# Two batches' leftover tokens are projected and transposed together in a kernel of attention, gated convolution and spectral mixing

## The chip, the cores and the metric

The kernel runs on one core of a Trainium2 chip. The metric is the device time of one execution in microseconds (us). A core has a matrix engine (TensorE, PE in the profile; its weight loads are the rows PEld), VectorE (DVE), ScalarE (ACT), GpSimd (POOL) and SyncE (SP), which issues the DMA transfers. Each engine runs its own list of instructions in order, and they wait for one another on semaphores.

## The reference

For 4 batches of 576 tokens and width 512 (8 heads of 64):

```python
scores = q @ k.T / 8                       # per head, 576 x 576
kth    = 32nd largest of each row
attn   = softmax(where(scores >= kth, scores, -1e9))
x      = concat_heads(attn @ v)            # 576 x 512

gate = sigmoid(causal 5-tap convolution of x along tokens, per channel)
x    = (gate * (x @ w_val)) @ w_out

u  = x + real(fft over tokens(fft over width(x)))
un = (u - mean(u)) / sqrt(var(u) + 1e-6)   # over the width
out = u + relu(un @ w_ch1) @ w_ch2         # 512 -> 2048 -> 512
```

## The kernel before

**Slots.** Attention is cut into 144 tiles: 4 batches of 4 pairs of heads, 9 tiles of 128 rows of scores to a pair (four to each head, and one that holds the last 64 rows of both). Slot s is one turn of a loop that every engine runs. In it PE makes the scores of tile s, transposes the probabilities of tile s-5 and, in every other slot, multiplies by v (`attend`, tile s-6). DVE finds the 32 largest of each row with eight passes over 576 columns, here called a search: the first half `search(s, 0)` (two MAX8 and two MATCH_REPLACE8) and the second `search(s, 1)` (two and one), for the tiles s-1 and s-2. ACT copies the scores, computes the exponentials of tile s-4 and copies the transposed probabilities.

**Steps.** Everything behind attention is a list of steps for each batch (`STEPS`, L109), which `steps_by_slot` (L160) spreads over the 36 slots that begin at slot 42, 78 and 114, by the costs of `COST`; the last batch has no attention beside it and takes one step a slot from slot 150 on. The steps of a batch are: `val` 0 to 7 (products with w_val; DVE multiplies them by the gate into `gv`), `zed` 2, 0, 1 and `seq` 0 to 2 (the two transforms), `proj` 0 to 4 (product with w_out, one for each tile of tokens; DVE's `make_u` adds the transform and takes mean and variance, GpSimd's `deviation` makes 1/sqrt, DVE's `normalise` makes `un`), `trn` 0 to 4 (PE transposes `un`, ACT copies it twice, as `un_hi` and back into `un`, GpSimd subtracts to get `un_lo`), then `ch0` and `ch1` 0 to 16 (for two groups of tokens: `hidden(f)` and behind it `sums(f-1)`).

**Where a step stands in its slot.** On every engine the first step of a slot's list stands before the second half of the slot's own work, the others behind it. On PE the order is scores, transposes, first step, `attend`, other steps. On DVE it is `search(s, 0)`, first step, `search(s, 1)`, other steps. On ACT the first step stands behind the exponentials, except a `ch0` step below 12.

**Tiles of tokens.** A batch has four tiles of 128 tokens and 64 left over, tile 4. The left over tokens of an even batch lie in rows 0 to 63 of `u[4]`, those of the odd batch behind it in rows 64 to 127. The matmuls of `ch1` take them together in the odd batch (`GROUPS`, L58), and the output is written from there for both. Before the change everything from `proj` 4 to `trn` 4 is done in each batch for itself: in the even batch with 64 rows, and in the odd one the product is made for 128 rows, of which 64 are used.

**Waits that the steps below name.** `zed` 2 waits before each quarter k for the gate products, the last of them for both parts of `val` 7. `project(2)` waits for the copy of `seq` 0, `transpose_un(n)` for `normalise(n)`, `hidden(b, 0, 0)` for `un_lo` of the first two tiles, `sums(b, 0, 0)` for all of `make_u`. The third and fourth buffers of w_ch2 and w_ch1 hold parts of w_out, so SP loads them again only when the last projection is done. In batches 0 and 2 the list puts `val` 6 and 7 into slots 45 and 117, `proj` 0 and 1 into 49 and 121, `seq` 1 and `proj` 2 into 50 and 122, `proj` 3 into 51 and 123, `trn` 0, `trn` 1 and `seq` 2 into 52 and 124, `proj` 4 and `ch0` 0 into 53 and 125. In batch 1, `val` 4 to 6 are in slot 80 and `val` 7 and `zed` 2 in slot 81.

Of the kernel before, what the change touches and what calls it, by code (L numbers as in the profile page):

```python
# [9 lines left out]
ALU = mybir.AluOpType  # L10
# [46 lines left out]

GROUPS = [[[0, 2], [1, 3]], [[0, 2], [1, 3, 4]]]  # L58
# [27 lines left out]

def hidden_bank(b, g, f):

    if g == 0:
        return 3 if f == 1 or f >= 12 and f % 2 == 0 else 2  # L90

    return 2 if (b % 2 == 0 or f == 1) and f % 2 else 3
# [13 lines left out]
TRN_BANK = [3, 2, 3, 3, 3]  # L106
# [9 lines left out]
NORM_AT = {("proj", 1): 0, ("proj", 2): 1, ("ch0", 1): 2, ("ch0", 4): 3, ("ch0", 7): 4}  # L116
COST = {"val": 2.2, "zed": 3.0, "seq": 2.6, "proj": 2.9, "trn": 0.6, "ch0": 3.1}
# [42 lines left out]
def steps_by_slot():  # L160

    out = {s: [] for s in range(ALL_TILES + ATTEND)}
    for b in range(B):
        steps = [(what, b, n) for what, n in STEPS]
# [16 lines left out]
def build(nc, qT, kT, v, w_val, conv_w, w_out, w_outT, w_ch1, w_ch2, feat, cosT, sinT, ident, out):  # L181
    with ExitStack() as ctx:
# [213 lines left out]
        def out_rows(b, r):  # L396

            return slice(0, LEFT) if r == NR - 1 and b % 2 == 0 else slice(0, P)

        def gv_cols(b, r):  # L400
            return slice(ROWS[r][0], ROWS[r][0] + out_rows(b, r).stop)
# [25 lines left out]
        with nc.Block() as block:  # L427

            @block.sync
            def _(sp):  # L430
# [49 lines left out]
                def load_w1(i):  # L480
                    if i % (2 * FC) == NB1 - 1:
                        sp.wait_ge(m_y, NR * (i // (2 * FC) + 1))
                    if i >= NB1:
                        sp.wait_ge(m_h, i - NB1 + 1)
                    sp.dma_start(w1_st[i % NB1][:, :, :, :].bitcast(F32), w1_split[i % FC]).then_inc(m_w1in[i % NB1], 16)

                def load_w2(i):
                    if i % (2 * FC) == NB2 - 1:
                        sp.wait_ge(m_y, NR * (i // (2 * FC) + 1))
# [73 lines left out]
            def _(pe):  # L563
# [129 lines left out]
                def sequence(b, g):  # L693
                    if g == 0:
                        pe.wait_ge(s_resid, 80)
                    elif g == 2:
                        pe.wait_ge(m_u, 2 * NR * b + 4)
# [12 lines left out]
                def project(b, r):  # L710
# [5 lines left out]
                    elif r == 3:  # L716
                        pe.wait_ge(m_u, 2 * NR * b + 2)
                    elif r == 4:
                        pe.wait_ge(m_u, 2 * NR * b + 8)

                    bank = mbank(PROJ_BANK[r])[out_rows(b, r), :]
                    for n, (x, h) in enumerate(((gv_hi, 0), (gv_hi, 1), (gv_lo, 0))):
                        for k in range(KC):
                            for c0, c1, w in w_out_half(b, k, h):
                                mm = pe.matmul(bank[:, c0:c1], x[:, k, gv_cols(b, r)], w, start=n + k == 0,  # L725
# [3 lines left out]
                def transpose_un(b, n):  # L729
                    r = LN[n]  # L730
                    pe.wait_ge(m_un, NR * b + n + 1)
                    if n == 0:
                        pe.wait_ge(m_u, 2 * NR * b + 6)
                    elif n == 1:
                        pe.wait_ge(m_abev, 3 * b + 2)
                    else:
                        pe.wait_ge(m_unT, 2 * (NR * b + n))
                        pe.wait_ge(m_hev, 2 * FC * b + 2)
                    m, at = ROWS[r][1], rows(b, r)
                    bank = mbank(TRN_BANK[n])  # L740
                    for k in range(KC):
                        mm = pe.transpose(bank[:, k * P:k * P + m], un[n % 2][at, k * P:k * P + P], id_sb[at, at])
                    mm.then_inc(m_tr, 1)

                def hidden(b, g, f):
                    i = (2 * b + g) * FC + f
                    if f == 0:
                        pe.wait_ge(m_unlo, NR * b + (NR if g else 2))
# [3 lines left out]
                    if g == 0 and f == 12:  # L752
                        pe.wait_ge(m_unT, 2 * NR * (b + 1))
# [7 lines left out]
                def sums(b, g, f):  # L761
# [3 lines left out]
                    if f == 0 and g == 0:  # L765
                        pe.wait_ge(m_u, 2 * NR * (b + 1))
# [48 lines left out]
            def _(act):  # L815
# [87 lines left out]
                def step(what, b, n):  # L903
# [13 lines left out]
                    elif what == "trn":  # L917
                        m = ROWS[LN[n]][1]
                        act.wait_ge(m_tr, NR * b + n + 1)
                        bank = mbank(TRN_BANK[n]).rearrange("p (k n) -> p k n", k=KC)[:, :, 0:m]  # L920
                        act.activation(un_hi[:, :, un_cols(b, LN[n])], bank, ACT.Copy).then_inc(m_unT, 1)
                        act.activation(un[n % 2][:, 0:KC * m].rearrange("p (k n) -> p k n", k=KC), bank,
# [19 lines left out]
                for s in plan:  # L942
# [7 lines left out]
                    first = any(what == "ch0" and n < 12 for what, b, n in plan[s][0:1])  # L950
# [28 lines left out]
            def _(dve):  # L979
# [94 lines left out]
                def make_u(b, r):  # L1074
                    g = [0, 0, 1, 1, 2][r]
                    at = rows(b, r)
# [28 lines left out]
                def step(what, b, n):  # L1105
                    if what == "val":
# [3 lines left out]
                        if b and n == 0:  # L1110
                            dve.wait_ge(m_y, NR * b)
# [9 lines left out]
                    if (what, n) in NORM_AT:  # L1121
# [22 lines left out]
                for s in plan:  # L1144
                    if due(s, RECIP) and unit_end(s - RECIP) is not None and s - RECIP >= POOL_RECIP:
                        reciprocal(s - RECIP)
                    search(s, 0)
                    for x in plan[s][0:1]:
# [10 lines left out]
                    for x in plan[s][1:]:  # L1159
# [3 lines left out]
            def _(pool):  # L1163
# [180 lines left out]
```

## Time and profile before

| | |
|---|---|
| median of 3 runs | 1044.3 us (1043.85 to 1046.93) |
| the profiled execution | 1048.86 us, of which the span of instructions is 1047.1 us |
| busy: PE, PEld | 965.9 us (92%), 826.2 us (79%) |
| busy: DVE, ACT, POOL | 842.2 us (80%), 645.5 us (62%), 406.9 us (39%) |
| mean granted clock of TensorE | 0.969 |

The profiled execution is one run and 4.6 us above the median. Busy is the union of the spans of an engine's instructions. The ends of matmuls are modelled, so the engine's real pace is read from the starts of its rows, and from the weight loads. A wait is put down to the instruction that came last by the profile.

### The profile page before, as it was taken

What the parts mean: (1) busy time and instruction counts of PE and PEld (TensorE: products, weight loads), DVE (VectorE), ACT (ScalarE), POOL (GpSimd) and SP (SyncE); (2) the same over time, 40 slices, a digit from 0 to 9 for tenths busy, and PEclk for the clock granted to TensorE, in tenths of its full rate; (3) what the DMA queues carried; (4) which work ended last, traced back from release to release, by engine and by line L of the source; (5) the groups of instructions that cost most, each with busy time, mean ns of one, the idle gap of its engine ahead of it and who ended that gap; (6) DMA issues with size and microseconds to landing.
All of it is one profiled execution on the core that took longest, in us unless ns stands there. A gap on an engine that the chain in (4) does not pass through costs nothing.

```text
span 1047.1 us, 20137 instructions
## 1 busy us (share of the span) xinstructions
PE 965.9 (92%) x6784; PEld 826.2 (79%) x6784; DVE 842.2 (80%) x1840; ACT 645.5 (62%) x1421; POOL 406.9 (39%) x543
## 2 busy tenths in 40 slices
PE   4877777899999999989999999989999999999997
PEld 3555566678888898778998898878889887888896
DVE  7999999999999999989999987898999973220000
ACT  5887787965777767556776566666786661132121
POOL 1674554544443333244342333244442222443221
PEclk9997868999999999999999999999999999999999
DMA  8565756550277777401877565410677676069873
GB/s 246 175 197 172 257 175 195 178 191 24 88 284 257 273 271 276 140 18 64 289 262 262 187 219 178 144 34 24 236 255 259 255 253 212 1 227 346 288 247 128
DMA packets 84549, 203.80 MB, mean 195 GB/s; under 512 B 9056, under 2 KB 30304, under 8 KB 84448
## 3 DMA queue, kind: packets, MB, share of 16 engines
q1 hardware_dynamic: 84128, 201.93, 56.6%
q8 instruction: 55, 0.90, 0.4%
q10 hardware_dynamic: 320, 0.59, 0.2%
q14 instruction: 46, 0.38, 0.1%
HBM read 178.89 MB, written 23.59 MB: 193 GB/s over the span
## 4 chain that ended last, share of the span: by engine, by line
PE 59%; DVE 28%; issue 9%; ACT 2%; POOL 1%; DMA 1%; SPq 0%; DVEq 0%; ACTq 0%; POOLq 0%
PE p_m L757 16%; PE p_m L774 15%; DVE rest L1007 13%; DVE top L996 11%; PE p_m L725 5%; PE p_t L605 5%; PE p_t L589 4%; PE p_s L575 4%; PE p_m L616 3%; PE p_m L706 3%; PE p_m L648 2%; DVE gate L1070 1%; DVE gv L1116 1%; PE p_t L609 1%; DMA w_st<-w_split 1%
## 5 line engine op out<-in xcount | busy, mean ns | idle before, releaser
L996 DVE MAX8 top<-rest 128x8 f32<-128x576 f32 x432 | 312.4, 753 | 0.1
L1272 POOL TENSOR_TENSOR hid_lo<-hid,hid_hi 128x256 fp32r<-128x256 f32 (+1 forms) x128 | 107.7, 842 | 299.2 <-ACT hid_hi L932 299.2
L1007 DVE MATCH_REPLACE8 rest<-top,rest 128x576 f32<-128x576 f32 x288 | 216.3, 751 | 0.0
L774 PE MATMUL p_m<-w_st,hid_hi 128*128 128x512 f32 x576 | 181.2, 396 | 3.1 <-DMA w_st<-w_split 1.8
L757 PE MATMUL p_m<-un_hi,w_st 128*128 128x256 f32 (+1 forms) x1024 | 164.3, 303 | 0.0
L838 ACT ACTIVATE s_sb<-p_s 128x576 f32<-128x576 f32 x144 | 93.0, 646 | 98.1 <-PE p_s L575 98.1
L757 PEld LDWEIGHTS p_m<-un_hi,w_st 128*128 128x128 f32 x1024 | 143.5, 188 | 5.6 <-issue 1.9
L931 ACT ACTIVATE hid<-p_m 128x256 f32<-128x256 f32 (+1 forms) x128 | 51.8, 405 | 129.2 <-PE p_m L757 128.3
L589 PE MATMUL p_t<-id_sb,prob 128*128 128x128 f32 x720 | 108.3, 282 | 24.2 <-ACT prob L856 23.9
L605 PE MATMUL p_t<-pT,v_sb 128*64 128x128 f32 (+1 forms) x1600 | 106.6, 284 | 24.3 <-ACT pT L864 24.3
L605 PEld LDWEIGHTS p_t<-pT,v_sb 128*64 128x64 f32 x1600 | 87.5, 146 | 49.0 <-ACT pT L864 30.0
L575 PE MATMUL p_s<-k_hi,q_st 128*128 128x288 f32 x320 | 108.4, 354 | 14.6 <-DVE q_st L1140 8.3
L856 ACT ACTIVATE prob<-prob,bias 128x576 f32<-128x576 f32 x144 | 111.8, 776 | 16.2
L774 PEld LDWEIGHTS p_m<-w_st,hid_hi 128*128 128x128 f32 x576 | 101.1, 188 | 19.8 <-POOL hid_lo L1272 2.2
L774 PE MATMUL p_m<-w_st,hid_lo 128*128 128x512 f32 x288 | 113.5, 394 | 0.0
L589 PEld LDWEIGHTS p_t<-id_sb,prob 128*128 128x128 f32 x720 | 87.1, 144 | 32.4 <-ACT prob L856 30.5
L996 DVE MAX8 top<-s_sb 128x8 f32<-128x576 f32 x144 | 109.7, 762 | 2.9 <-ACT s_sb L838 2.8
L850 ACT ACTIVATE prob<-s_sb,top 128x576 f32<-128x576 f32 x144 | 111.0, 771 | 0.0
L1007 DVE MATCH_REPLACE8 rest<-top,s_sb 128x576 f32<-128x576 f32 x144 | 108.1, 751 | 0.0
L864 ACT ACTIVATE pT<-p_t 128x640 f32<-128x640 f32 x144 | 101.3, 703 | 6.3 <-PE p_t L589 6.3
L1103 DVE TENSOR_TENSOR u<-p_m,u 128x512 f32<-128x512 f32 x18 | 11.5, 685 | 112.9 <-PE p_m L774 112.8
L575 PE MATMUL p_s<-k_lo,q_st 128*128 128x288 f32 x320 | 93.6, 307 | 0.0
(118 smaller groups left out, 1655.8 us busy)
## 6 DMA issues: line engine op xcount, KB each, us to landing
w_st<-w_split SPq DMA_DIRECT2D x256, 512.0 KB, 4.8
w_split<-w_st SPq DMA_DIRECT2D x32, 512.0 KB, 3.4
k_raw<-kT SPq DMA_DIRECT2D x62, 144.0 KB, 3.0
q_raw<-qT SPq DMA_DIRECT2D x60, 144.0 KB, 2.9
u<-w_ch SPq DMA_DIRECT2D x32, 256.0 KB, 4.0
v_sb<-v SPq DMA_DIRECT2D x16, 256.0 KB, 3.0
w_st<-wout_split SPq DMA_DIRECT2D x16, 256.0 KB, 3.9
out<-u SPq DMA_DIRECT2D x16, 256.0 KB, 2.5
```

What stands on the lines that cost most here:

```text
L575: mm = pe.matmul(p_s[:, o, 0:HALF_S], q_st[h][p % 2][:, cols], k[:, o * HALF_S:o * HALF_S + HALF_S], start=n == 0, stop=n == len(parts) - 1)
L589: mm = pe.transpose(p_t[:, c * P:c * P + P], prob[t % 3][:, c * P:c * P + P], id_sb[:, :])
L605: pe.matmul(p_o[D * h:D * h + D, 0, 0:n], v_sb[p % 2][:, c, D * h:D * h + D], pT[tt % 3][:, c, c0:c0 + n], start=c == 0, stop=c == NCH - 1 ...
L757: mm = pe.matmul(mbank(hidden_bank(b, g, f), n), w1_st[i % NB1][:, w, k, :], x[:, k, at:at + n], start=part + k == 0, stop=part + k == KC + 1)
L774: mm = pe.matmul(mbank(j), h[i % 2][:, P * j:P * j + P], w2_st[i % NB2][:, w, :], start=f == 0 and part == 0, stop=f == FC - 1 and part == 2)
L838: act.activation(s_sb[t % NS][:, :].rearrange("p (o n) -> p o n", o=2), p_s[:, :, 0:HALF_S], ACT.Copy, scale=SCALE).then_inc(s_copy, 1)
L850: act.activation(prob[t % 3][:, 0:S], s_sb[t % NS][:, :], ACT.Prelu, bias=kth, scale=-1.0, alpha=1.0 / BIG).then_inc(s_drop, 1)
L856: act.activation(prob[t % 3][:, 0:S], prob[t % 3][:, 0:S], ACT.Exp, bias=bias[t % NK][:, :], scale=-BIG, accum_out=psum_row[:, t % NK:t % ...
L864: act.activation(pT[t % 3][:, :, :].rearrange("p c n -> p (c n)"), p_t[:, 0:SP], ACT.Copy).then_inc(s_pT, 1)
L996: found = dve.max(top[t % NK][:, 8 * n:8 * n + 8], (rest[t % 2] if n else s_sb[t % NS])[:, :])
L1007: chained(dve.match_replace(rest[t % 2][:, :], top[t % NK][:, 8 * n:8 * n + 8], (rest[t % 2] if n else s_sb[t % NS])[:, :], LOWEST), t)
L1272: pool.tensor_tensor(hid_lo[i % 2][:, 0:width(b, g)], hid[:, 0:width(b, g)], hid_hi[i % 2][:, 0:width(b, g)].bitcast(F32), ALU.subtract).t ...
```

## The change

- The even batches have no `proj` 4 and no `trn` 4 any more, and `deviation` and `normalise` of tile 4 are gone there too. `plus_minus` of `seq` 2 writes its result straight into rows 0 to 63 of `u[4]`.
- In the odd batch `make_u` of tile 4 first adds the product of the even batch's 64 rows to them, one DVE operation on 64x512 more. Statistics, deviation, normalising, transposes, copies and `un_lo` of tile 4 are made for all 128 rows there.
- In even batches `trn` 0 stands before `proj` 3, with the two banks of PSUM for `trn` 0 and 1 exchanged. `hidden` alternates its banks from f = 10 instead of 12.
- `deviation` of tile 3 stands behind `un_lo` of `trn` 1 on GpSimd, for all batches, and not at `proj` 3.
- DVE does the first step of a slot ahead of `search(s, 0)` if it is a `val` from 4 on.
- ACT does `ch1` 0 ahead of the exponentials if it is the first step of its slot (slots 66 and 138 after the change).
- The counts of semaphores follow (`us`, `outs`), and SP waits for four projections in an even batch.
- With 56 steps in place of 58, `steps_by_slot` gives the even batches other slots: of batch 0, slot 50 `seq` 1; 51 `proj` 2, `trn` 0, `proj` 3; 52 `trn` 1, `seq` 2; 53 `ch0` 0; 54 `ch0` 1 and 2. Slots 42 to 49 and 71 to 77 keep their steps, and so do all of batch 1 and 3; batch 2 has the pattern of batch 0, 72 slots later.

```diff
-TRN_BANK = [3, 2, 3, 3, 3]
+TRN_BANK = [[2, 3, 3, 3], [3, 2, 3, 3, 3]]
...
+LAST_TILE = [("proj", NR - 1), ("trn", NR - 1)]
+def steps_of(b):
+    if b % 2:
+        return STEPS
+    steps = [x for x in STEPS if x not in LAST_TILE]
+    steps.remove(("trn", 0))
+    steps.insert(steps.index(("proj", 3)), ("trn", 0))
+    return steps
...
 def load_w1(i):
     if i % (2 * FC) == NB1 - 1:
-        sp.wait_ge(m_y, NR * (i // (2 * FC) + 1))
+        sp.wait_ge(m_y, outs(i // (2 * FC) + 1))
...
 def transpose_un(b, n):
-    pe.wait_ge(m_un, NR * b + n + 1)
-    if n == 0:
-        pe.wait_ge(m_u, 2 * NR * b + 6)
-    elif n == 1:
+    pe.wait_ge(m_un, outs(b) + n + 1)
+    if n < 2 and TRN_BANK[b % 2][n] == PROJ_BANK[2]:
+        pe.wait_ge(m_u, us(b) + 6)
+    elif n < 2:
         pe.wait_ge(m_abev, 3 * b + 2)
...
-first = any(what == "ch0" and n < 12 for what, b, n in plan[s][0:1])
+first = any(what == "ch0" and n < 12 or (what, n) == ("ch1", 0) for what, b, n in plan[s][0:1])
...
 def make_u(b, r):
...
     y = mbank(PROJ_BANK[r])
+    at, made = slice(0, P), us(b) + 2 * (r + 1)
+    if r == NR - 1:
+        at, made = rows(b, r), us(b + 1)
+        early = rows(b - 1, r)
+        dve.tensor_tensor(u[r][early, :], y[early, :], u[r][early, :], ALU.add).then_inc(m_u, 1)
...
-    if (what, n) in NORM_AT:
+    if (what, n) in NORM_AT and outs(b) + NORM_AT[what, n] < outs(b + 1):
         normalise(b, NORM_AT[what, n])
...
+    ahead = int(any(what == "val" and n >= KC for what, b, n in plan[s][0:1]))
+    for x in plan[s][0:ahead]:
+        step(*x)
     search(s, 0)
-    for x in plan[s][0:1]:
+    for x in plan[s][ahead:ahead + 1]:
         step(*x)
     search(s, 1)
...
 def plus_minus(b, g):
...
+    if g == 2 and b % 2 == 0:
+        if b:
+            pool.wait_ge(m_put, 16 * puts(b))
+        to = u[NR - 1][at, :]
+        pool.tensor_tensor(to[:, 1:NCOS - 1], a, bb, ALU.subtract).then_inc(m_pm, 1)
+        pool.tensor_tensor(to[:, DM - 1:NCOS - 1:-1], a, bb, ALU.add).then_inc(m_pm, 1)
+        for n in (0, NCOS - 1):
+            pool.tensor_copy(to[:, n:n + 1], ab[at, n:n + 1]).then_inc(m_pm, 1)
+        return
...
-elif what == "proj" and n < NR - 1:
+elif what == "proj" and n < 3:
     deviation(b, n)
 elif what == "trn":
...
+    if n == 1:
+        deviation(b, 3)
```

## Rows read from the trace of the kernel before

**Rows 1.** Stretches: length, busy of PE, PEld, DVE, ACT, POOL, clock, DMA share, GB/s

```profile
232.00:234.00 2.00, 2.00 (x7) 1.63 (x6) 2.00 (x5) 2.00 (x5) 1.29 (x2) 0.50 0.00 0
...
265.00:444.00 179.00, 176.78 (x1396) 154.12 (x1394) 177.48 (x388) 128.85 (x294) 63.91 (x83) 1.00 0.67 231
...
450.00:453.00 3.00, 3.00 (x9) 2.45 (x8) 2.96 (x9) 2.88 (x7) 1.91 (x2) 0.50 0.00 0
...
602.00:660.00 58.00, 58.00 (x405) 51.76 (x404) 45.67 (x97) 37.91 (x82) 17.23 (x19) 1.00 0.57 198
...
971.00:1041.00 70.00, 69.43 (x342) 61.83 (x342) 1.29 (x2) 13.95 (x32) 16.16 (x16) 1.00 0.63 224
```

**Rows 2.** Timeline of PE: start, us, operation [idle before <-releaser]; `zed` 2

```profile
229.85 0.66 PE L682 MATMUL p_m<-wfeat,gv 128*64 128x257 f32 x4 [2.00 <-DVE gv L1116]
...
444.56 0.65 PE L682 MATMUL p_m<-wfeat,gv 128*64 128x257 f32 x4 [0.44 <-DVE gv L1116]
448.13 0.65 PE L682 MATMUL p_m<-wfeat,gv 128*64 128x257 f32 x4 [2.91 <-DVE gv L1116]
...
688.75 1.12 PE L682 MATMUL p_m<-wfeat,gv 128*64 128x257 f32 x4 [2.97 <-DVE gv L1116]
```

**Rows 3.** Timeline of DVE, slots 120 to 123: its idle times (batch 0 has their like)

```profile
704.85 0.15 DVE L1054 TENSOR_SCALAR rinv<-psum_row 128x1 f32<-128x1 f32 x1 [0.47 <-ACT prob L856]
...
708.68 0.43 DVE L1084 TENSOR_TENSOR u<-p_m,pm 128x257 f32<-128x257 f32 x1 [0.69 <-PE p_m L725]
...
713.20 0.43 DVE L1084 TENSOR_TENSOR u<-p_m,pm 128x257 f32<-128x257 f32 x1 [0.80 <-PE p_m L725]
...
720.80 0.43 DVE L1084 TENSOR_TENSOR u<-p_m,pm 128x257 f32<-128x257 f32 x1 [0.64 <-PE p_m L725]
...
723.50 0.55 DVE L1097 TENSOR_SCALAR un<-u,mv,rstd 128x512 f32<-128x512 f32 x1 [0.99 <-POOL rstd L1249]
```

**Rows 4.** Timeline of DVE, slot 81: from its first search pass to `gv`

```profile
444.75 0.76 DVE L996 MAX8 top<-s_sb 128x8 f32<-128x576 f32 x1
...
447.52 0.55 DVE L1116 SCALAR_TENSOR_TENSOR gv<-gate,p_m 128x63 f32<-128x63 f32 x2
```

**Rows 5.** Timeline of DVE, slot 117: its start, second half of search, `gv`

```profile
683.00 0.76 DVE L996 MAX8 top<-s_sb 128x8 f32<-128x576 f32 x1
...
686.11 1.41 DVE L996 MAX8 top<-rest 128x8 f32<-128x576 f32 x2
...
688.15 0.54 DVE L1116 SCALAR_TENSOR_TENSOR gv<-gate,p_m 128x63 f32<-128x63 f32 x2
```

**Rows 6.** Timeline of DVE, slot 125: `make_u` of tile 4 and what follows

```profile
738.55 0.41 DVE L1084 TENSOR_TENSOR u<-p_m,pm 64x257 f32<-64x257 f32 x1
...
740.14 1.38 DVE L996 MAX8 top<-rest 128x8 f32<-128x576 f32 x2
```

**Rows 7.** Groups of instructions, forms apart: xcount, busy us, mean ns, idle before

```profile
L1103 DVE TENSOR_TENSOR u<-p_m,u 128x512 f32<-128x512 f32 x18 | 11.5, 685 | 112.9 <-PE p_m L774 112.8
...
L1097 DVE TENSOR_SCALAR un<-u,mv,rstd 64x512 f32<-64x512 f32 x4 | 3.4, 843 | 10.1 <-POOL un_lo L1263 10.1
```

**Rows 8.** Timeline of PE, slots 124 and 125: `attend`, `trn` 1, `proj` 4, `hidden`

```profile
726.53 1.31 PE L605 MATMUL p_t<-pT,v_sb 128*64 128x128 f32 x20 [0.36 <-ACT pT L864]
...
727.99 0.66 PE L742 MATMUL p_m<-id_sb,un 128*128 128x128 f32 x4
...
732.95 0.48 PE L725 MATMUL p_m<-w_out,un_hi 128*64 128x512 f32 x1
...
735.83 1.11 PE L757 MATMUL p_m<-un_hi,w_st 128*128 128x256 f32 x8
```

**Rows 9.** Timeline of PE: `trn` 4 of batch 2 and the scores behind it

```profile
778.40 0.46 PE L742 MATMUL p_m<-id_sb,un 64*128 64x64 f32 x4
778.79 0.40 PE L575 MATMUL p_s<-k_hi,q_st 128*128 128x288 f32 x1
```

**Rows 10.** Timeline of PE: `val` 6 of batch 2, slot 117

```profile
677.55 1.90 PE L648 MATMUL p_m<-x_new,wslot 128*128 128x257 f32 x8
```

More of the change, by code:

```diff
@@ L85, in un_cols @@
     return slice(c0, c0 + ROWS[r][1])
+TRANSPOSED = [10, 12]
 def hidden_bank(b, g, f):
     if g == 0:
-        return 3 if f == 1 or f >= 12 and f % 2 == 0 else 2
+        return 3 if f == 1 or f >= TRANSPOSED[b % 2] and f % 2 == 0 else 2
     return 2 if (b % 2 == 0 or f == 1) and f % 2 else 3
@@ L163, in steps_by_slot @@
     for b in range(B):
-        steps = [(what, b, n) for what, n in STEPS]
+        steps = [(what, b, n) for what, n in steps_of(b)]
         start = NT * (b + 1) + ATTEND
@@ L394, in folded, with tile_cols @@
             return gate[:, c, o * HALF + P * m:o * HALF + P * m + P]
[L396 to L401, printed above, removed]
+        def tile_cols(r):
+            return slice(ROWS[r][0], ROWS[r][0] + P)
         def w_out_half(b, k, h):
@@ L751, in hidden @@
                         pe.wait_ge(m_hev, hidden_before(i) + 1)
-                    if g == 0 and f == 12:
-                        pe.wait_ge(m_unT, 2 * NR * (b + 1))
+                    if g == 0 and f == TRANSPOSED[b % 2]:
+                        pe.wait_ge(m_unT, 2 * outs(b + 1))
                     at, n = HALF * g, width(b, g)
@@ L917, in step @@
                     elif what == "trn":
[L918 to L922, printed above, removed]
+                        act.wait_ge(m_tr, outs(b) + n + 1)
+                        bank = mbank(TRN_BANK[b % 2][n]).rearrange("p (k n) -> p k n", k=KC)
+                        act.activation(un_hi[:, :, tile_cols(LN[n])], bank, ACT.Copy).then_inc(m_unT, 1)
+                        act.activation(un[n % 2][:, :].rearrange("p (k n) -> p k n", k=KC), bank,
                                        ACT.Copy).then_inc(m_unT, 1)
@@ L1158, in _ @@
                         conv(b, c, part, taps)
-                    for x in plan[s][1:]:
+                    for x in plan[s][ahead + 1:]:
                         step(*x)
@@ L1244, in deviation @@
                 def deviation(b, r):
[L1245 to L1249 removed]
+                    pool.wait_ge(m_mv, outs(b) + r + 1)
+                    pool.tensor_scalar(rstd[:, r, 0:1], mv[:, r, 1:2], EPS_VAR, None, ALU.add).then_inc(m_var, 1)
+                    pool.wait_ge(m_var, outs(b) + r + 1)
+                    pool.tensor_tensor(rstd[:, r, 1:2], rstd[:, r, 0:1], power[:, 0:1], ALU.pow).then_inc(m_rstd, 1)
                 def step(what, b, n):
@@ L1273, in step @@
                                            hid_hi[i % 2][:, 0:width(b, g)].bitcast(F32), ALU.subtract).then_inc(m_hlo, 1)
-                        if g == 0 and n == 1:
+                        if g == 0 and n == 1 and b % 2:
                             deviation(b, NR - 1)
```

64 lines of the change are left out of this document (28 added, 36 removed).

## The prediction

> **What bounds the kernel now.** I read first the busy time by stretch, then every idle time of DVE and of PE in their timelines, and asked at each idle time which of the two had been late. From 230 us on both look full: in 265 to 444 us PE is busy 176.8 of 179 us and DVE 177.5 [rows 1]. The weight loads are busy 154.1 of these 179 us, 86%, against 61.8 of 70, 88%, in the last stretch, where nothing but PE works [rows 1]. So PE really works at nearly its full pace, with DVE as full beside it. PE runs one to two slots ahead of DVE, and that lead lets neither stop for the other except at few places. These places tell which engine the end depends on.
>
> PE stops for DVE before `zed` 2: 2.0 us at 229.9, 0.4 and 2.9 us at 444.6 and 448.1, 3.0 us at 688.8 [rows 2]. It needs the gate products of `val` 6 and 7, and DVE makes them behind its search. DVE stops for PE or for what hangs on PE in the slots of `proj`: 0.47, 0.69, 0.80 and 0.64 us, and 0.99 us for GpSimd's deviation, in batch 2 [rows 3]; batch 0 has the same five within 0.03 us. In 602 to 660 us DVE is busy only 45.7 of 58 us while PE is never idle [rows 1]. So the path to the end goes: DVE up to 230; PE up to the `proj` steps of batch 0; DVE to 448, without an idle time of note; PE through batch 1 to about 659; DVE through `val` to 689; PE from 689 to the end. A saving counts if it lies on this path, on that engine.
>
> **Gate products first.** In slot 81 DVE starts its search at 444.75 and `val` 7 follows at 447.52 [rows 4]. The change puts it in front: 2.77 us earlier. In slots 45 and 117 `val` 6 is the first step and `val` 7 the second; they are now done before `search(s, 0)` and between the halves, so `val` 7 is earlier by the second half, 688.15 - 686.11 = 2.04 us [rows 5]. DVE does the same work in another order. PE gets 2.04 us earlier into `zed` 2 of batches 0 and 2 and, by this part alone, 2.77 us in batch 1.
>
> **DVE in batch 0.** With PE 2.04 us earlier, y of `proj` 0 and 1 and the exponentials come before DVE needs them: the idle times of 0.47, 0.69 and 0.80 us sum to 1.96, less than 2.04. `proj` 2 moves from behind slot 50's search to slot 51, so that DVE reaches it half a search (2.77 us) later, and PE only by a slot's scores and transposes; the idle time of 0.64 goes too. The 0.99 us for the deviation stays. That is 2.60 us of idle time gone from DVE. Of `make_u` for tile 4, 740.14 - 738.55 = 1.59 us go [rows 6]; `normalise` on 64 rows took 0.84 us in the mean of four, on 128 rows 0.55, taken as 0.60 since one of the four was long [rows 3, 7]. Sum for batch 0, on DVE: 2.60 + 1.59 + 0.60 = 4.8 us. With the 2.77 us of slot 81 `zed` 2 of batch 1 starts 7.6 us earlier. PE arrives there 2.04 us earlier and without `proj` 4 and `trn` 4 (2.88 and 0.39 us, below), together 5.3 us. It stood 3.35 us for DVE before [rows 2] and stands 3.35 - 7.6 + 5.3 = 1.1 us now: DVE stays the later one, and what PE saves in this batch is hidden.
>
> **Batch 1.** PE's work is the same but for four transposes with 128 instead of 64 columns, some 0.05 us. DVE has one addition more; the nearest row, on twice the rows and the same columns, took 0.69 us [rows 7]. It lies between 468 and 602 us, where PE leads and DVE's later idle time (12.3 us of 602 to 660 [rows 1]) covers it; were the cover gone, it would cost those 0.69 us, and I keep 0 to 0.7. The 7.6 us are carried to 659.
>
> **Batch 2.** DVE's `val` 7 gives 2.04 us at 689. From there PE's path counts. `proj` 4 took 735.83 - 732.95 = 2.88 us and `trn` 4 0.39 us [rows 8, 9]. That would be 5.3 us, if nothing new makes PE wait. What can is `trn` 1. It waits for `normalise(1)`, which follows `make_u` of `proj` 2, and this now stands in slot 123 behind another first half of a search. Worked out: `normalise(1)` began at 723.50; without the idle times before it (1.96 + 0.64) and with 2.77 us of search and two small operations of 0.15 us [rows 3] more before it, it begins at 723.97 and ends at 724.5. PE's `trn` 1 began at 727.99, so it can start 3.5 us earlier, not 5. Between it and `hidden` lay 7.84 us, of which 2.88 are `proj` 4; `attend`, 1.46 us, which stood before it, now stands behind it [rows 8]. So `hidden(0)` starts at 724.5 + 7.84 - 2.88 + 1.46 = 730.9, 4.9 us earlier than the 735.83 of before, and with `trn` 4 it is 5.3 us. That the two ways agree means that `trn` 1 is nearly just in time: PE waits there 0 to 1 us, and what PE gains more before it is lost in front of it. `hidden(0)` itself needs `un_lo` of `trn` 1: ACT's copies stand behind an exponential, GpSimd's subtraction behind them, by my sum at 728.8, which leaves 2 us. `deviation` of tile 3 behind it hides in GpSimd's idle time, and `normalise` of tile 3 comes five slots later.
>
> **The last batch** has its order. `deviation` out of the way lets `un_lo` come about 1 us sooner, but PE did not wait for it. Its loads of weights start again when `proj` 4 ends, as before, so that stretch moves as one. Cost of the wider `trn` 4 and of the addition: 0 to 0.5 us, taken as 0.1.
>
> **Sum.** 7.6 + 5.3 - 0.1 = 12.8 us off the profiled execution's 1048.86, which gives 1036.1. Off the median of 1044.3 it gives 1031.5.
>
> **A rule against the trace: the clock.** The granted clock is 0.50 in 450 to 453 us, the lower level of 1.2 GHz, behind the waits of 444.6 and 448.1, and in 232 to 234 us behind that of 229.9 [rows 1, 2]; at 688.8 the four matmuls of `zed` 2 took 1.12 us against 0.65 [rows 2]. A low stretch of 3 us costs about 1.5 us against full speed. In batch 1 PE now stands some 1.1 us in place of 3.35. Whether the clock then stays at 2.4 GHz no row decides. The forecast leaves the low stretch in batch 1, and takes no gain in 0 and 2, where DVE or `trn` 1 swallows it.
> The Trainium skill (TensorE: Matmul & The Clock Gate, "What's actually happening") says that the throttled clock is the default and that activity releases it; by it shorter waits would keep the higher level, and the time would be about 1030.0 instead of 1031.5. The trace agrees as far as it shows the low level only behind such waits in this part.
>
> **Rivals.**
> 1. *The clock stays up in batch 1.* For it: the wait shrinks to a third, and PE carries batch 1 alone. Against it: the wait of 2.0 us at 229.9 was enough for a fall. Time: 1031.5 - 1.5 to 2 = 1029.5 to 1030, down to 1027 if other small waits go with it.
> 2. *The even batches get new waits on PE.* `proj` 4 was 2.88 us of PE work between `trn` 1 and `hidden(0)`, which hid the way from `un` through PE, ACT and GpSimd. If my 2 us of slack are not there, PE waits 1 to 3 us in each even batch, and in batch 2 it counts, perhaps with a low clock of 1.5 us behind it: 1033 to 1038.
> 3. *The change gives nothing measurable.* That would be if DVE's order, not PE's work, carried batches 1 and 2 as well. DVE's 12.3 us of idle time before 660 [rows 1] speak against it. Time: within 3 us of 1044.
> 4. *Slower: DVE stands before `val`.* DVE now does a product ahead of its search, and must wait if PE is not done with it; before, 2.77 us of search covered that. Six slots have it (44, 45, 80, 81, 116, 117). If PE has no lead there, DVE stands 2.77 us in each, 16.6 us in all, against 12.8 gained: 1044.3 + 3.8 = 1048. It decides from the point at which PE's product ends later than DVE's slot begins. In slot 117 it ended at 679.45 and DVE began at 683.00 [rows 5, 10], 3.5 us to spare. Since PE gains at least what DVE gains, I hold it for unlikely.
>
> **How the numbers follow.** Forecast (1030.5 to 1033): 0.44. Rival 1: 0.22. Rival 2: 0.22. Rival 3: 0.06. Rival 4: 0.06. About 0.3%, 3.1 us, is what a measurement of this kernel tells from no change. The range that holds 8 in 10 leaves out the two last cases and little more: 1027 to 1039. Faster by over 0.3% 0.88, within 0.3% 0.06, slower 0.06.
>
> **What would show it.** In the profile after: `zed` 2 of batches 0, 1 and 2 near 228, 440.5 and 679 us; PE's idle time before them below 0.5, 1.5 and 1.5 us; no idle time of DVE for y in batches 0 and 2; 18 statistics and 18 `normalise` in place of 20; `hidden(0)` of batch 2 about 12.5 us earlier than 735.8; a short wait before `trn` 1 for `normalise`. Wrong would be: `zed` 2 of batch 1 later than 442, which refutes the part on DVE; `hidden(0)` waiting for `un_lo`; idle DVE at the head of slots 44 or 80; a tail from the end of attention that is longer than before.

## The result, and the profile after

The kernel after took 1039.38 us in the median of 7 runs (1038.66 to 1042.03), the one before 1046.02 us in 7 runs (three of them gave the 1044.3 us from which the forecast was made): a ratio of the means of 0.9943, with a 95% interval of 0.9925 to 0.9960. So 6.6 us went between the medians, of 12.8 forecast. The time is 0.4 us above the range's upper end; the forecast of 1031.5 would be 1033.2 from the 1046.0 of before, and misses by 6 us from there too. The profiled execution took 1041.2 us, with a span of 1039.4, 7.7 less than the 1047.1 of before.

Where the forecast was short is seen when the span is cut at the starts of `zed` 2's last gate product in batches 1 and 2 and at `zed` 2's first in batch 3:

| Stretch | before | after | change | forecast |
|---|---|---|---|---|
| start to `zed` 2 of batch 1 | 448.1 | 444.2 | -3.9 | -7.6 |
| to `zed` 2 of batch 2 | 240.6 | 237.2 | -3.4 | -2.0 |
| to `zed` 2 of batch 3 | 201.9 | 203.3 | +1.4 | -3.3 |
| to the end | 156.5 | 154.8 | -1.7 | +0.1 |

These are the rows of TensorE in the kernel after that answer to [rows 2]; there is no idle time before `zed` 2 of batch 0 any more. The prediction had named `zed` 2 of batch 1 later than 442 us as what refutes its part on DVE, and it starts at 444.2.

```profile
444.20 0.66 PE L703 MATMUL p_m<-wfeat,gv 128*64 128x257 f32 x4 [1.20 <-DVE gv L1138]
...
681.37 0.65 PE L703 MATMUL p_m<-wfeat,gv 128*64 128x257 f32 x4 [0.93 <-DVE gv L1138]
...
683.68 1.11 PE L610 MATMUL p_t<-id_sb,prob 128*128 128x128 f32 x4 [0.93 <-ACT prob L875]
```

The waits for `gv` are 1.2 and 0.9 us in place of 3.4 and 3.0. Behind the third row, a wait for exponentials, a low clock remains. The stretches of the kernel after, with the columns of [rows 1]; the third number from the end is the granted clock:

```profile
230.00:233.00 3.00, 3.00 (x18) 2.68 (x17) 3.00 (x7) 3.00 (x7) 1.97 (x2) 1.00 0.00 0
277.00:281.00 4.00, 4.00 (x18) 3.38 (x16) 4.00 (x9) 2.52 (x6) 0.73 (x1) 0.57 0.86 247
449.00:452.00 3.00, 3.00 (x19) 2.79 (x18) 2.96 (x9) 3.00 (x7) 1.18 (x1) 1.00 0.00 0
684.00:687.00 3.00, 3.00 (x11) 2.54 (x10) 3.00 (x7) 3.00 (x7) 1.96 (x2) 0.50 0.03 5
```

Against [rows 1], the clock stays at 1.00 at 230 and at 449, and there is a new low stretch at 277. The next view explains this one and most of the missing gain: TensorE's waits from the first `proj` of batch 2 to that of batch 3.

```profile
PE p_t L610 <- ACT prob L875: 2.8, 2, 2.1
PE p_m L761 <- DVE un L1119: 1.2, 1, 1.2
PE p_t L626 <- ACT pT L883: 0.9, 2, 0.5
PE p_m L793 <- POOL hid_lo L1308: 0.7, 2, 0.5
```

With a fifth of 0.2 us they sum to 5.8 us; before, the same stretch had 2.5 us. What is new are 2.1 us for exponentials in slot 126 and 1.2 us for `normalise` before `trn` 1. The rows of TensorE there:

```profile
721.32 0.66 PE L761 MATMUL p_m<-id_sb,un 128*128 128x128 f32 x4 [1.16 <-DVE un L1119]
...
727.58 1.19 PE L776 MATMUL p_m<-un_hi,w_st 128*128 128x256 f32 x8
...
731.88 0.77 PE L610 MATMUL p_t<-id_sb,prob 128*128 128x128 f32 x5 [2.10 <-ACT prob L875]
```

ACT's timeline, first of the kernel after, then of before, shows why:

```profile
729.35 0.38 ACT L949 ACTIVATE hid<-p_m 128x256 f32<-128x256 f32 x1 [0.78 <-PE p_m L776]
729.62 0.38 ACT L950 ACTIVATE hid_hi<-p_m 128x256 fp32r<-128x256 f32 x1
...
730.07 0.77 ACT L869 ACTIVATE prob<-s_sb,top 128x576 f32<-128x576 f32 x1
730.96 0.77 ACT L875 ACTIVATE prob<-prob,bias 128x576 f32<-128x576 f32 x1
```

```profile
734.90 0.78 ACT L856 ACTIVATE prob<-prob,bias 128x576 f32<-128x576 f32 x1
...
737.51 0.39 ACT L931 ACTIVATE hid<-p_m 128x256 f32<-128x256 f32 x1 [1.74 <-PE p_m L757]
```

In slot 125 of before, `proj` 4 was the first step and `ch0` 0 the second, so ACT made the exponentials while TensorE was in `proj` 4 [rows 8], and copied `hidden(0)` behind them. With `proj` 4 gone, `ch0` 0 is the first step, and ACT's rule puts the copies of a first `ch0` step ahead of the exponentials. ACT then stands until `hidden(0)` is made, the exponentials come behind it, and TensorE, which has only scores in between, waits for them. The removed 2.9 us of work had been the cover of this chain. Batch 0 has the same wait, and the low clock of 277 behind it:

```profile
276.16 0.77 PE L610 MATMUL p_t<-id_sb,prob 128*128 128x128 f32 x5 [2.04 <-ACT prob L875]
```

The second wait comes from a row that is longer than its like. VectorE's `normalise` before `trn` 1, and the GpSimd row beside it:

```profile
719.78 1.48 DVE L1119 TENSOR_SCALAR un<-u,mv,rstd 128x512 f32<-128x512 f32 x1 [0.99 <-POOL rstd L1284]
```

```profile
719.71 1.27 POOL L1298 TENSOR_TENSOR un_lo<-un,un_hi 128x512 fp32r<-128x512 f32 x1
```

The same operation took 0.55 us before [rows 3]. In the new order `un_lo` of `trn` 0 is GpSimd's next operation behind the deviation that lets `normalise` start, so that the two start within 0.07 us of each other in both even batches.

### The profile page after: what moved, and what is told of

It is laid out like the page before. It is cut to its first block, busy times and chain, and to the rows that moved or that the text cites. A ratio compares the mean times of both kernels' runs of the same rounds, so it can differ in the third digit from the quotient of the medians.

```text
span 1039.4 us, 20032 instructions
## 1 busy us (share of the span) xinstructions
PE 960.1 (92%) x6744; PEld 823.1 (79%) x6744; DVE 841.0 (81%) x1832; ACT 644.9 (62%) x1417; POOL 404.0 (39%) x537
## 4 chain that ended last, share of the span: by engine, by line
PE 58%; DVE 25%; issue 10%; POOL 3%; ACT 3%; DMA 1%; SPq 1%; DVEq 0%; ACTq 0%; POOLq 0%
PE p_m L776 17%; PE p_m L793 16%; DVE rest L1025 12%; DVE top L1014 10%; PE p_t L626 5%; PE p_t L610 4%; PE p_s L596 4%; PE p_m L746 4%; PE p_m L637 3%; PE p_m L727 2%; PE p_m L669 2%; POOL hid_lo L1308 1%; PE p_t L630 1%; DMA k_raw<-kT 1%; DVE gate L1088 1%
## 5 line engine op out<-in xcount | busy, mean ns | idle before, releaser
L1025 DVE MATCH_REPLACE8 rest<-top,rest 128x576 f32<-128x576 f32 x288 | 214.1, 743 | 0.0
```

The costliest lines, as they stand in the source:

```text
L1025: chained(dve.match_replace(rest[t % 2][:, :], top[t % NK][:, 8 * n:8 * n + 8], (rest[t % 2] if n else s_sb[t % NS])[:, :], LOWEST), t)
```

## The experiments

Each has 5 or 6 runs (e4 has 12), and the kernel before was timed with each of three groups of them (e1 to e4, e5 to e8, e9 to e12): its medians were 1046.75, 1047.02 and 1047.23 us. Ratios are of means, to the kernel before of the same group. The last columns are stretches of one profiled execution between the first `proj` matmuls of two batches; the last one is followed by 142.7 to 143.1 us in every kernel but before, which had 144.5. One execution can lie some us off its kernel's median (e9's 3.6 above, e5's 2.7 below); in e2 and e9 some 2 us of that fall ahead of 200 us, where no edit reaches. A difference of under 1 us between stretches is not to be leaned on.

| Kernel | median us | ratio (95%) | batch 0-1 | 1-2 | 2-3 |
|---|---|---|---|---|---|
| before | 1046.0 | | 218.1 | 240.6 | 197.2 |
| after | 1039.4 | 0.9943 (0.9925-0.9960) | 215.5 | 240.1 | 197.3 |
| e1 val ahead alone | 1039.2 | 0.9925 (0.9909-0.9941) | 213.6 | 237.8 | 197.5 |
| e2 exponentials before ch0 0 | 1035.3 | 0.9896 (0.9879-0.9912) | 212.4 | 237.5 | 195.8 |
| e3 slots kept | 1040.7 | 0.9948 (0.9932-0.9964) | 213.8 | 238.3 | 199.5 |
| e4 val behind | 1050.0 | 1.0017 (0.9998-1.0036) | 218.4 | 242.3 | 198.8 |
| e5 removal, order of before | 1037.6 | 0.9917 (0.9893-0.9941) | 212.9 | 238.1 | 195.6 |
| e6 e2, lone steps too | 1034.6 | 0.9899 (0.9871-0.9926) | 211.5 | 237.6 | 195.0 |
| e7 e2, deviation back | 1039.8 | 0.9941 (0.9918-0.9963) | 215.1 | 238.0 | 198.0 |
| e8 e2, trn 0 behind proj 3 | 1034.6 | 0.9898 (0.9873-0.9924) | 212.5 | 237.9 | 196.1 |
| e9 e6 and e8 | 1031.9 | 0.9859 (0.9841-0.9878) | 210.9 | 237.9 | 195.5 |
| e10 e6, un_lo behind normalise | 1031.2 | 0.9853 (0.9832-0.9873) | 210.5 | 237.6 | 194.0 |
| e11 e5, lone steps | 1034.9 | 0.9883 (0.9865-0.9902) | 212.6 | 237.6 | 194.6 |
| e12 e1, lone steps | 1038.4 | 0.9912 (0.9896-0.9927) | 213.3 | 238.2 | 196.3 |

The cuts are rows of TensorE like these, of before, of after and of e10:

```profile
246.72 0.48 PE L725 MATMUL p_m<-w_out,un_hi 128*128 128x512 f32 x1
...
464.81 0.48 PE L725 MATMUL p_m<-w_out,un_hi 128*128 128x512 f32 x1
...
705.40 0.48 PE L725 MATMUL p_m<-w_out,un_hi 128*128 128x512 f32 x1
...
902.61 0.47 PE L725 MATMUL p_m<-w_out,un_hi 128*128 128x512 f32 x1
```

```profile
243.72 0.48 PE L746 MATMUL p_m<-w_out,un_hi 128*128 128x512 f32 x1
...
459.21 0.48 PE L746 MATMUL p_m<-w_out,un_hi 128*128 128x512 f32 x1
...
699.35 0.48 PE L746 MATMUL p_m<-w_out,un_hi 128*128 128x512 f32 x1
...
896.63 0.47 PE L746 MATMUL p_m<-w_out,un_hi 128*128 128x512 f32 x1
```

```profile
243.39 0.48 PE L746 MATMUL p_m<-w_out,un_hi 128*128 128x512 f32 x1
...
453.94 0.48 PE L746 MATMUL p_m<-w_out,un_hi 128*128 128x512 f32 x1
...
691.52 0.48 PE L746 MATMUL p_m<-w_out,un_hi 128*128 128x512 f32 x1
...
885.54 0.47 PE L746 MATMUL p_m<-w_out,un_hi 128*128 128x512 f32 x1
```

**Which half of the change gives the gain: e1 and e4.** e1 is the kernel before with `val` ahead and nothing else, e4 the kernel after without it.

```diff
 # e1, in the kernel before
+ahead = int(any(what == "val" and n >= KC for what, b, n in plan[s][0:1]))
+for x in plan[s][0:ahead]:
+    step(*x)
 search(s, 0)
-for x in plan[s][0:1]:
+for x in plan[s][ahead:ahead + 1]:
 # e4, in the kernel after
-ahead = int(any(what == "val" and n >= KC for what, b, n in plan[s][0:1]))
+ahead = 0
```

> The kernel before, with one part of the change: DVE does a val step from 4 on ahead of its search where that is the first step of its slot. Theory A (work and order both count; new waits on PE ate most of what the removed work gave): zed 2 of batch 0 and 2 starts 2.0 us sooner against DVE's slots, that of batch 1 2.8 us, the low clock stretch of batch 0 goes; 3 to 5 us less than before, and the rest of the change's 6 us is what is left of the removed work. Theory B (the removed projection and transposes lie beside the path and give nothing; the order of val is the whole gain): 6 us less than before, ratio 0.994.

> The changed kernel with DVE's val steps behind the first half of the search, as in the kernel before. Theory A: loses 3 to 5 us against the changed kernel, so 1 to 3 us better than the kernel before. Theory B: no faster than the kernel before.

e1 took 1039.23 us, 7.5 less than before and the same as with the whole change. Its wait for `gv` in batch 1 was 0.80 us at 444.26, and no low clock is left between 205 us and the last matmuls. e4 took 1050.02 us in the median, but its 12 runs lie in two groups, five at 1044.1 to 1045.8 us and seven at 1049.5 to 1051.9, on both sides of the 1046.75 of before; why they part is not shown, and the profiled one (1050.83) is of the longer seven. The interval of its ratio holds 1, so the rest of the change without `val` ahead gives nothing that can be measured, and whether it costs some is open. TensorE of e4:

```profile
688.94 1.12 PE L703 MATMUL p_m<-wfeat,gv 128*64 128x257 f32 x4 [2.97 <-DVE gv L1138]
...
739.61 1.33 PE L610 MATMUL p_t<-id_sb,prob 128*128 128x128 f32 x5 [2.10 <-ACT prob L875]
```

Both waits are there, and behind both the row is long: the four products took 1.12 us for 0.65, the transposes 1.33 for 0.77, at the lower clock. In the kernel as it was changed, the order of VectorE is the whole measurable gain.

**Is the wait in slots 54 and 126 the loss: e2.**

```diff
-first = any(what == "ch0" and n < 12 or (what, n) == ("ch1", 0) for what, b, n in plan[s][0:1])
+first = any(what == "ch0" and 0 < n < 12 or (what, n) == ("ch1", 0) for what, b, n in plan[s][0:1])
```

> The changed kernel, except that ScalarE does its exponentials ahead of ch0 0 (in slots 53 and 125, where ch0 0 now is the first step of its slot). Theory A: PE's wait of 2.1 us for the exponentials at 276 and 732 us goes; 2 to 4 us less than the changed kernel, 1035 to 1037. Theory B: PE's waits there are covered, within 1 us of the changed kernel.

1035.32 us, 4.1 less than the kernel after. TensorE's wait fell from 2.10 to 0.67 us, and the low clock of 277 is gone. The two intervals lie apart, so this wait, with what it brings behind it, is most of what was missing. ACT and TensorE of e2:

```profile
727.24 0.77 ACT L875 ACTIVATE prob<-prob,bias 128x576 f32<-128x576 f32 x1
...
728.02 0.36 ACT L949 ACTIVATE hid<-p_m 128x256 f32<-128x256 f32 x1
```

```profile
728.16 0.77 PE L610 MATMUL p_t<-id_sb,prob 128*128 128x128 f32 x5 [0.67 <-ACT prob L875]
```

**The slots of before: e3 and e5.** In e3 the even batches keep every slot of before, with empty places for `proj` 4 and `trn` 4, and `trn` 0 stands behind `proj` 3. e5 is e3 without ACT's new rule for `ch1` 0.

```diff
 # e3, in the kernel after
-steps = [x for x in STEPS if x not in LAST_TILE]
-...
+return [("no_" + x[0], x[1]) if x in LAST_TILE else x for x in STEPS]
 # e5, in e3
-first = any(what == "ch0" and n < 12 or (what, n) == ("ch1", 0) for what, b, n in plan[s][0:1])
+first = any(what == "ch0" and n < 12 for what, b, n in plan[s][0:1])
```

> The changed kernel, but every step of the even batches stands in the slot and place that it has in the kernel before, with empty places where proj 4 and trn 4 were, and trn 0 behind proj 3: the work is removed and nothing is moved up. Theory A: neither the wait before trn 1 (1.3 us) nor that for the exponentials (2.1 us) nor the collision of normalise with un_lo appears, and DVE keeps its lead behind slot 53; 3 to 6 us less than the changed kernel. Theory B: as the changed kernel, within 1 us. A third outcome, slower than the changed kernel by 1 us or more, would say that the new spread over the slots is a gain in itself.

> The kernel after, with the slots of before in the even batches (as in e3: empty places stand where proj 4 and trn 4 of tile 4 were, trn 0 behind proj 3) and without ACT's new rule for ch1 0, so that against e1 only the removal of the even batches' tile 4 is left. e3 had two waits on ACT of 2.3 to 2.6 us ahead of the transposes of the slots with ch1 0 alone (350.93, 804.35), the second with 3.4 us at clock 0.50 behind it. Theory A (the removed work counts once no new wait stands in its place): 2.2 us of VectorE's work in batch 0 and 3.3 us of TensorE's in batch 2 are gone against e1, which had 1039.2, so 1034 to 1037, and about 4 us under e3 (1040.7), with the waits at 351 and 804 gone. Theory B (the removed work lies beside the path): the same as e1, 1038.5 to 1040, 1 to 2 us under e3 for the low clock alone.

e3 took 1040.66 us, no less than the kernel after. The slot list alone is not the cause: the wait at `ch0` 0 is down to 0.67 us in e3 (at 726.97), but in its list `ch1` 0 is alone in its slot, and ACT's new rule makes the same wait there, 2.11 us at 350.93 and 2.39 at 804.35. TensorE of e3, then the stretch behind it at clock 0.50:

```profile
804.35 0.90 PE L606 MATMUL p_t<-id_sb,prob 128*128 128x128 f32 x3 [2.39 <-ACT prob L871]
```

```profile
804.00:807.00 3.00, 2.65 (x13) 2.65 (x14) 3.00 (x7) 2.12 (x6) 0.00 (x0) 0.50 0.30 117
```

e5 took 1037.59 us, with both waits down to 0.67 us: 3.1 less than e3. Against e1 it is only the removal of tile 4: 1.6 us less in the medians, whose intervals overlap, and 2.4 us less between the first `proj` of batch 0 and that of batch 3 (646.5 against 648.9), where e5's profiled execution was one of its two shortest. Theory A had hoped for 2 to 5; it is between the two, and by e5 alone the removed work is not shown to be worth anything.

**Lone steps: e6, e11, e12.** ACT puts the exponentials first also where a `ch0` or `ch1` step is alone in its slot. e6 adds this to e2, e11 to e5, e12 to e1 (in e11 and e12 for `ch0` alone, and with e2's `0 < n`).

```diff
-first = any(...)
+first = any(...) and (len(plan[s]) > 1 or s >= ALL_TILES)
```

> e2 (exponentials ahead of ch0 0) with ACT's exponentials also ahead of any ch0 or ch1 step that is the only step of its slot. In e2 the waits of 0.5 to 0.9 us ahead of the transposes in the slots with one step stayed. Theory A: each is a hole that TensorE doesn't get back in batch 2, some 1 to 2 us there and as much less in batch 0: 1033 to 1035 against 1035.3 for e2. Rival: where the copy of hidden comes later, the sums of the slot behind wait in place of the transposes, by the 0.5 us of two more exponentials each: 1035 to 1037.

> e5 (the slots of before, tile 4 of the even batches left to the odd ones, ch1 0 behind the exponentials) with ACT's exponentials ahead of any ch0 step that is alone in its slot. e5 had waits of 0.67 to 0.72 us ahead of the transposes of six such slots in batches 0 and 2. Theory A: 1 to 2 us less than e5 (1037.6) in each of the two: 1033.5 to 1036. Theory B (the order on ACT doesn't matter beside the removed work): 1037 to 1038.5.

> The kernel before with val ahead (e1, 1039.2) and ACT's exponentials ahead of any ch0 step that is alone in its slot, so with all of tile 4's work in the even batches. With e1, e5 and e11 it makes a square of two edits. e1 had four waits of 0.67 to 0.71 us ahead of transposes in batches 0 and 2. Theory A (they add up): 1 to 2 us less than e1, 1037 to 1038.5, and e11 1 to 3 us below this kernel, the removed work. Rival: the order on ACT was the whole gain of e6, and this kernel is at 1034 to 1036 like it, so that the removed work is worth nothing even there.

Medians 1034.56, 1034.90 and 1038.42 us, each 0.8 to 2.7 less than the kernel it was made from, and each time with overlapping intervals; the profiled stretches say 1.6, 1.7 and 1.2 us. So what the order of lone steps is worth is not shown by any one of them. What the square shows better is the removed work: e11 is 3.5 us below e12 (1033.3 to 1037.7 against 1036.2 to 1039.1 us; the intervals of their ratios just overlap), and its stretches are 0.7, 0.6 and 1.7 us shorter. The rival of e12, that the order was all, fell.

**The deviation, put at nothing: e7.**

```diff
 # in e2
-elif what == "proj" and n < 3:
+elif what == "proj" and n < 4:
     deviation(b, n)
 ...
-if n == 1:
-    deviation(b, 3)
```

> e2 with the deviation of tile 3 back at proj 3 on GpSimd, in all batches. It is two short operations; the prediction put the move at nothing. If that holds: within 1 us of e2 (1035.3). Rival (it was moved because it waits for the mean and variance of tile 3 ahead of un_lo of trn 1): un_lo of trn 0 and 1 come 1 to 2 us later, hidden 0 of the batches 0 and 2 waits for them, and its time is 1036.5 to 1038.5, with new TensorE waits at about 275 and 728 that end with GpSimd's un_lo.

1039.83 us, 4.5 more than e2: the rival was right, and its price too low by a second consequence. TensorE of e7:

```profile
726.32 1.22 PE L776 MATMUL p_m<-un_hi,w_st 128*128 128x256 f32 x8 [0.86 <-POOL un_lo L1298]
...
739.04 1.22 PE L776 MATMUL p_m<-un_hi,w_st 128*128 128x256 f32 x8 [1.39 <-DMA w_st<-w_split]
```

The deviation of tile 3 stands on GpSimd until 722.64 for VectorE's statistics, with `q_st` and `un_lo` of `trn` 1 behind it. GpSimd of e7 and then of e2:

```profile
725.00 1.27 POOL L1298 TENSOR_TENSOR un_lo<-un,un_hi 128x512 fp32r<-128x512 f32 x1
...
728.28 1.41 POOL L1201 TENSOR_TENSOR k_lo<-k_raw,k_hi 128x576 fp32r<-128x576 f32 x1
```

```profile
721.49 1.27 POOL L1298 TENSOR_TENSOR un_lo<-un,un_hi 128x512 fp32r<-128x512 f32 x1 [1.10 <-ACT un L940]
...
726.06 1.43 POOL L1201 TENSOR_TENSOR k_lo<-k_raw,k_hi 128x576 fp32r<-128x576 f32 x1
```

`un_lo` is 3.5 us later and `hidden(0)` waits for it. `k_lo` is 2.2 us later, and SP loads the next keys into its buffer only then (its queue starts at 729.72 us in e7, at 727.52 in e2); the loads of weights stand behind these in the same queue and start at 733.40 instead of 731.19. So a fourth `hidden` waits 1.39 us for its weights, and 1.85 us in batch 0. e7 is e2 with this one move undone: the change needs it.

**The slow `normalise`: e8, e9, e10.** e8 is e2 and e9 is e6 with `trn` 0 behind `proj` 3. e10 is e6 with one wait more.

```diff
 # e8, e9
-steps.remove(("trn", 0))
-steps.insert(steps.index(("proj", 3)), ("trn", 0))
 # e10
 pool.wait_ge(m_unT, 2 * (outs(b) + n + 1))
+if n == 0:
+    pool.wait_ge(m_un, outs(b) + 2)
```

> e2 with trn 0 of the even batches back behind proj 3. In the kernel after, TensorE waits 1.2 to 1.3 us before trn 1 for VectorE's normalise of it, which took 1.48 us instead of 0.55 while GpSimd's un_lo of trn 0 ran beside it. With trn 0 behind proj 3 the two no longer meet. Theory A: the wait of 1.3 us before trn 1 goes in batches 0 and 2 and normalise is back at 0.5 to 0.6 us: 1033.5 to 1035 against 1035.3. Rival: the waits move to trn 0 or to hidden 0, whose un_lo then comes later (less than one slot between them): 1035 to 1037.5.

> e6 and e8 together: the kernel after, with ACT's exponentials ahead of a step that is alone in its slot and ahead of ch0 0, and trn 0 of the even batches behind proj 3. From the first projection of batch 0 to that of batch 3, e2 takes 645.7 us, e6 644.1 and e8 646.4. Theory A (each wait taken away is time): 1033 to 1035, like e6, since e8 without the wait of 1.2 us before trn 1 was no shorter than e2. If the wait before trn 1 were worth its length in each even batch: 1031 to 1033.

> e6 with one wait more on GpSimd: un_lo of trn 0 waits until VectorE's normalise of trn 1 is done, so that the two no longer run at the same time. In e6 and after both start as soon as GpSimd's deviation of that tile is done, and normalise took 1.48 us where it takes 0.53 to 0.55 alone. Theory (the shared time is what makes normalise long): it is 0.53 to 0.6 us long in this kernel in batches 0 and 2, and the wait before trn 1, 1.16 us at 715, is 0.9 us shorter. Rival (normalise is long for another reason, as a first operation behind a pause of VectorE): it stays at 1.4 to 1.5 us. The time: un_lo of trn 0 begins 0.6 us later, with 1.1 us of free time on GpSimd behind it; 1032.5 to 1034.5, no more than 2 us under e6 (1034.6).

e8 took 1034.61 us, 0.7 less than e2, which can't be told from none. The wait before `trn` 1 is gone, but `normalise` is as long as ever, since GpSimd now starts `q_st` where `un_lo` was, and one slot later TensorE stands for weights, which e2 does not. TensorE, VectorE and GpSimd of e8:

```profile
734.95 1.22 PE L774 MATMUL p_m<-un_hi,w_st 128*128 128x256 f32 x8 [0.68 <-DMA w_st<-w_split]
```

```profile
715.15 1.48 DVE L1117 TENSOR_SCALAR un<-u,mv,rstd 128x512 f32<-128x512 f32 x1 [0.99 <-POOL rstd L1282]
```

```profile
715.08 1.72 POOL L1194 TENSOR_TENSOR q_st<-q_raw,q_st 64x512 fp32r<-64x512 f32 x2
```

e10 keeps GpSimd off. VectorE, GpSimd and TensorE of e10:

```profile
711.95 0.55 DVE L1119 TENSOR_SCALAR un<-u,mv,rstd 128x512 f32<-128x512 f32 x1 [0.99 <-POOL rstd L1284]
```

```profile
712.64 1.28 POOL L1300 TENSOR_TENSOR un_lo<-un,un_hi 128x512 fp32r<-128x512 f32 x1 [0.73 <-DVE un L1119]
```

```profile
712.55 0.66 PE L761 MATMUL p_m<-id_sb,un 128*128 128x128 f32 x4 [0.23 <-DVE un L1119]
```

`normalise` is back at 0.55 us and TensorE waits 0.23 us instead of 1.16, in both even batches. Between the first `proj` of batch 0 and that of batch 3 e10 takes 642.2 us, e6 644.1: 1.9 us, which is twice 0.93. The length of `normalise` is shown with this; its price is less sure. The median is 1031.21 us, 3.3 below e6, more than I had expected, and the intervals of the two just overlap; e6 was timed in another group. e9 does not separate the two and still took 1031.94 us, which can't be told from e10. With a ratio of 0.9853 to the kernel before, e10 beats both the kernel before and the one after.

## Why the prediction was wrong

**The sign, the bound and `val` ahead were right.** The gate products come earlier as worked out: e1 alone gives 7.5 us where the terms for it sum to 6.8 (1.96 of idle time, 2.77 and 2.04), and 7.0 in the three profiled stretches. The sum had nothing in it for the low clocks behind the waits, which are gone in e1. VectorE has no idle time before a `val` in any of the six slots, so rival 4 fell. Rival 3 fell too: 6.6 us were measured, and VectorE stands idle before 660 us as it did. That the order on VectorE is the whole gain of the change as made is not what it had named; the removed work gives nothing there because new waits stand in its place.

**Batch 0: the step that failed is the sum of 4.8 us on VectorE.** From the start of slot 46 to that of slot 81 VectorE took 214.0 us, and 214.8 before: 0.7 us less. Slot 81 of after begins with the gate products of `val` 7, the last two of the three in this row, 0.46 us ahead of its search at 444.07:

```profile
443.28 0.87 DVE L1138 SCALAR_TENSOR_TENSOR gv<-gate,p_m 128x257 f32<-128x257 f32 x3
```

The work went, but 2.60 us less idle time had been worked out, and there was 0.9 more (4.7 us for 3.8). New are 0.43, 0.43, 1.65 and 0.75 us, all behind TensorE's waits of 1.13 and 2.04 us at 265.65 and 276.16; the longest:

```profile
327.00 0.17 DVE L1072 TENSOR_SCALAR rinv<-psum_row 128x2 f32<-128x2 f32 x1 [1.65 <-ACT prob L875]
```

In e2, where the second of these waits is 0.68 us, the idle time is 2.1 us and the stretch 211.7; in e10, where neither is over 0.7 us, they are 1.0 and 208.7. So it is TensorE's waits that cost VectorE its gain. A smaller part is operations that took longer than their like, as `normalise` does beside GpSimd's: rows of VectorE over 0.05 us longer than the median of their form sum to 3.0 us in these slots before, and to 4.5 after. The forecast took `normalise` at 0.60 us, "since one of the four was long"; two of the four were (1.44 us at 525.38 and 0.87 at 937.46), and e10 shows such a length to be the sign of a mechanism and not noise. By the stretches of the table, e10's batch 0 is 7.6 us shorter than before's (210.5 against 218.1), 5.0 below the kernel after.

**Batch 2: the step that failed is "if nothing new makes PE wait. What can is `trn` 1."** The work removed there was right, 2.88 and 0.39 us, and so were the 2 us of slack of `hidden(0)`: `un_lo` ended at 725.04 and `hidden(0)` started at 727.58, without a wait. What the list left out is the transposes of the next slot, which wait for ACT's exponentials. The waits between the first `proj` of batches 2 and 3 grew by 3.3 us, 2.1 of them there, and the stretch stayed as it was (197.3 against 197.2). In e2, with this wait at 0.67 us, it is 1.4 us shorter than before's, and in e10, with waits of before's size (2.7 us for 2.5), 3.2 us. Rival 2 had half of the mechanism, `proj` 4 as a cover, but looked for the wait at `hidden(0)`, behind `un_lo`, and its 1033 to 1038 us end below the 1039.4 measured. I had read in the code that a `ch0` step as first step of its slot goes ahead of the exponentials, and had not asked which step becomes the first when `proj` 4 is gone.

**The wait before `trn` 1** was put at 0 to 1 us and was 1.16, with `normalise` 0.93 us longer than in the sum; in e10, with `normalise` at 0.55, the wait is 0.23.

**The deviation** was put at nothing. Undone, it costs 4.5 us. The forecast asked only whether it hides where it now stands, and not what it would have held up where it stood. My reading of the code is that before, with `trn` 0 behind `proj` 3, nothing that was urgent stood behind it on GpSimd; no run tests that apart.

**Idle times for y** in slots 120 to 123 were said to go. Three of the four stayed (0.41, 0.69 and 0.80 us at 698.81, 702.63 and 707.15), since TensorE lost its advance in batch 2 to the wait at 683.68 and the low clock behind it: in e2, with 0.40 us in that place and the clock at 1.00, all four are gone.

**The clock.** Rival 1 came true in batch 1: with a wait of 1.2 us in place of 3.35, the low stretch of 450 is gone, and the stretch from `zed` 2 of batch 1 to that of batch 2 is 3.4 us shorter where 2.0 were forecast. In batch 0 it is gone at 232 and came at 277. The Trainium skill (TensorE: Matmul & The Clock Gate, "What's actually happening") has activity release the throttle, and the trace agrees in batch 1; no run shows why the wait of 2.04 us at 276 was followed by a fall and that of 2.10 us at 731.88 was not.

**The end** was forecast unchanged and is 1.7 us shorter. Before had there a wait of 1.77 us for weights at 971.54, and of all the others only e4 has one in that place, of 0.62. One profiled execution can't say whether this is the kernel's or the execution's; e1, with the same order in the last batch, has the shorter end too. It stays open, as does the share of it in the medians.

## What to carry to other kernels

Work that is taken out of one engine was a cover for chains through others: name the chain that runs beside it (here scores, ACT's copy, exponentials, transposes), and ask after every removal which step now stands first in its place of the order. A rule of order that fits one list of steps must be looked at again for each new list. And an operation whose duration is bimodal in the trace should be followed to what runs beside it before its mean goes into a sum.

## What the runs showed of the hardware

Some of VectorE's operations take longer while GpSimd works beside them, and others do not. `normalise` of 128x512 takes 0.53 to 0.55 us, and 1.48 when a GpSimd subtraction of 1.27 us starts 0.07 us ahead of it. The mean of its group is 767 ns in the kernel after and 657 in e10:

```profile
L1119 DVE TENSOR_SCALAR un<-u,mv,rstd 128x512 f32<-128x512 f32 x18 | 13.7, 767 | 13.6 <-POOL un_lo L1298 9.7 <-POOL rstd L1284 4.0
```

```profile
L1119 DVE TENSOR_SCALAR un<-u,mv,rstd 128x512 f32<-128x512 f32 x18 | 11.7, 657 | 13.6 <-POOL un_lo L1300 9.7 <-POOL rstd L1284 4.0
```

The scaling into `rinv` (0.16 us, up to 1.07 in the kernel after) and the convolution's steps on `gate` (0.82, up to 1.86) show such lengths too, though no run took GpSimd away from them. Of the search passes (four MAX8 and three MATCH_REPLACE8 to a tile, seven and not eight) none does: all 576 MAX8 of the kernel after take 0.73 to 0.76 us. Nor does taking the statistics, 0.69 to 0.70 us, though it too has only operands in SBUF, nor the additions that read PSUM, 0.41 to 0.43. The Trainium skill (SBUF — State Buffer, "Who interferes with whom") says that the two engines share a pair of ports that is locked for a whole instruction by whichever comes first. The trace agrees in part: `normalise`, begun at 719.78, ended at 721.26, 0.28 us after GpSimd's operation beside it (719.71 and 1.27 us more), so that at least its end had to wait for that. That the lock holds for the whole instruction the trace doesn't show, since alone `normalise` takes 0.55 us and not 0.28, and spans on GpSimd are rough.
